# Asking for the next step's columns before the step's piece of w1, in a linear-attention and mixture-of-experts kernel

## The reference

```python
for t in range(S):                              # attention, B=4, H=8, S=768, D=48
    cur = einsum('bhd,bhe->bhde', u * k_t, v_t)
    y[:, :, t] = einsum('bhd,bhde->bhe', r_t, state + cur)
    state = w * state + einsum('bhd,bhe->bhde', k_t, v_t)
...
logits = x @ phi                                # mixture: x is 3072 x 384, 32 slots, 8 experts
slot_input = softmax_over_tokens(logits).T @ x
h = maximum(slot_input[e] @ w1[e], 0); slot_out[e] = h @ w2[e]      # w1[e] 384 x 1024
x = softmax_over_slots(logits) @ slot_out
...
h = x @ w_in; g = h * sigmoid(1.702 * h); out = g @ w_out           # 384 -> 2048 -> 384
```

## Time and profile before

| | |
|---|---|
| median of 3 runs | 385.01 us (383.77 to 385.17) |
| the profiled execution | 383.42 us, span 381.6 us |
| TensorE's granted clock | 0.999 of full |
| busy: TensorE, VectorE, ScalarE, POOL | 371.2, 233.2, 186.6, 98.2 us |
| DMA moved | 63.57 MB |
| attention stage | about 7 to 121 us |
| loop, chunks 1 to 4, on SyncE | 18.6 to 89 us |

### The profile page before, as it was taken

One profiled execution on the slowest core, in us unless ns is written; L12 is line 12 of the kernel. 1 busy time (PEld: TensorE's weight loads), 2 busy tenths in 40 slices (PEclk: granted clock), 3 DMA queues, 4 the chain that ended last, 5 costly groups with the idle time before them and its releaser, 6 DMA issues.

```text
span 381.6 us, 9077 instructions
## 1 busy us (share of the span) xinstructions
PE 371.2 (97%) x3198; PEld 290.7 (76%) x3198; DVE 233.2 (61%) x431; ACT 186.6 (49%) x398; POOL 98.2 (26%) x114
## 2 busy tenths in 40 slices
PE   6989999999999999999999999999999999999996
PEld 5877787877876344487888888888888888888885
DVE  8958697877783201687755556555555555555550
ACT  1234454445445241668565546455645564465451
POOL 6998888888671100100000000000000000000000
PEclk9999999999999999999999999999999999999999
DMA  7789999999999999600020002000200020002002
GB/s 287 269 313 395 398 391 397 400 392 375 391 336 413 342 394 413 254 0 2 1 82 3 0 2 82 0 0 0 82 0 0 0 82 0 0 5 78 0 2 82
DMA packets 21655, 63.57 MB, mean 167 GB/s; under 512 B 3073, under 2 KB 6674, under 8 KB 21250
## 3 DMA queue, kind: packets, MB, share of 16 engines
q1 hardware_dynamic: 20864, 63.09, 43.3%
q10 hardware_dynamic: 770, 0.19, 0.2%
HBM read 58.55 MB, written 4.72 MB: 166 GB/s over the span
## 4 chain that ended last, share of the span: by engine, by line
PE 94%; POOL 2%; DMA 2%; issue 1%; ACT 1%; DVE 0%; POOLq 0%; DVEq 0%; ACTq 0%
PE bank L651 11%; PE bank L653 11%; PE bank L652 11%; PE bank L392 6%; PE pair L651 6%; PE pair L652 6%; PE pair L653 6%; PE pair L441 6%; PE bank L638 4%; PE pair L429 3%; PE pair L412 3%; PE bank L600 3%; PE bank L462 3%; PE bank L580 2%; PE bank L471 2%; PE bank L453 2%
## 5 line engine op out<-in xcount | busy, mean ns | idle before, releaser
L946 DVE TENSOR_TENSOR gf<-bank,sg 128x512 f32<-128x512 f32 x72 | 49.8, 691 | 58.2 <-ACT sg L1155 58.0
L1155 ACT ACTIVATE sg<-bank 128x512 f32<-128x512 f32 x72 | 42.9, 598 | 70.6 <-PE bank L638 70.6
L651 PE MATMUL bank<-glo,whi 128*128 128x512 f32 x190 | 73.9, 389 | 0.0
L653 PE MATMUL bank<-ghi,wlo 128*128 128x512 f32 x190 | 73.9, 389 | 0.0
L652 PE MATMUL bank<-ghi,whi 128*128 128x512 f32 x190 | 73.9, 389 | 0.0
L957 DVE TENSOR_TENSOR glo<-gf,ghi 128x512 fp32r<-128x512 f32 x96 | 66.3, 691 | 0.3
L1161 ACT ACTIVATE ghi<-gf 128x512 fp32r<-128x512 f32 x95 | 59.4, 625 | 1.8 <-DVE gf L946 1.7
L652 PEld LDWEIGHTS bank<-ghi,whi 128*128 128x128 f32 x190 | 35.7, 188 | 7.4
L653 PEld LDWEIGHTS bank<-ghi,wlo 128*128 128x128 f32 x190 | 35.7, 188 | 7.4
L651 PEld LDWEIGHTS bank<-glo,whi 128*128 128x128 f32 x190 | 35.7, 188 | 7.4
L789 DVE TENSOR_TENSOR rks<-rkb,bank 112x512 f32<-112x512 f32 x48 | 30.8, 683 | 12.1 <-PE pair L429 7.1
(11 more groups left out here) (183 smaller groups left out, 510.4 us busy)
## 6 DMA issues: line engine op xcount, KB each, us to landing
ring<-w SPq DMA_DIRECT2D x24, 512.0 KB, 5.9
rkb<-rk SPq DMA_DIRECT2D x23, 512.0 KB, 5.9
krb<-kr SPq DMA_DIRECT2D x24, 384.0 KB, 5.0
ring<-w SPq DMA_DIRECT2D x4, 1536.0 KB, 13.8
ring<-w SPq DMA_DIRECT2D x8, 768.0 KB, 9.1
vb<-v SPq DMA_DIRECT2D x24, 192.0 KB, 5.0
out<-ob SPq DMA_DIRECT2D x18, 256.0 KB, 2.1
ring<-win SPq DMA_DIRECT2D x3, 1024.0 KB, 15.7
```

Of the source, the lines that this page charges most:

```text
L651: pe.matmul(o, w_hi, lo, start=(f == 0), stop=False)
L653: pe.matmul(o, w_lo, hi, start=False, stop=(f == KF - 1)).then_inc(prod_ps, 1)
L946: dve.tensor_tensor(gf[:, f % 2, :], bank[f % 4][:, :], sg[:, f % 2, :], ALU.mult).then_inc(gf_ok, 1)
L1155: act.activation(sg[:, f % 2, :], bank[f % 4][:, :], ACT.Sigmoid, scale=1.702).then_inc(sg_ok, 1)
```

## The change

In SyncE's `step` the line that asks for the next step's columns stands before the line that asks for the pieces of w1. Nothing else changes: the same requests, waits and buffers, and every other engine has the same instructions in the same order.

```diff
                 load_kr(c, b)
                 load_v(c, b)
-                load_w1(first, count)
                 if not (is_last(c) and b == B - 1):
                     load_rk(*following(c, b))
+                load_w1(first, count)
```

## The result

The change makes the kernel slower by a little: 386.23 us median of 14 runs (384.54 to 387.28) against 384.31 us for the kernel before, 14 runs taken beside them (383.34 to 386.26). The ratio is 1.0040, with a 95% interval of 1.0022 to 1.0058; that is +0.8 to +2.2 us, while the two medians are 1.9 us apart. I had forecast no change, with 385.0 us. The measured median lies within the stated range, but the two kernels differ beyond their scatter, and the forecast of no change is wrong.

A forecast was written before the change was run, and what follows sets the result against it. TensorE was taken to bound the loop, with the DMA close behind. The terms rk, w1, kr and dry queue summed to 0 (bounds -2.6 and about +0.5), giving a median of 385.0 us, range 383.4 to 386.6.

The forecast's parts named there:

- TensorE bounds the loop; the DMA has 0.75 us to spare a chunk: Attention loop, chunk 2: TensorE needs 18.65 us, the DMA 17.9 us for 7.08 MB at 396 GB/s.
- rk's issue does not move, it lands 1.3 us earlier, and no wait for it was on the path: Steady loop: rk still waits for VectorE's buffer, one w1 piece less lies ahead; gain 0, bounded by 2.6 us.
- w1 later costs 0 by itself: Loop: a w1 piece goes out some 2 us later; 14 us of cover before TensorE reads w1, cost 0.
- The issue of kr just fits: Step with two w1 pieces: kr could issue at 90.35, its buffer came free at 90.46; cost 0 to 0.1 us on SyncE.
- In the queue kr has the same bytes ahead of it as before, so it lands as before, provided that the queue never ran dry: Loop requests behind rk and w1: kr's landing stays unchanged if the queue never empties; cost 0.
- 0.2 us in all, bounds 0 and 0.5: Transfer time lost in the loop: a few dry moments of about 0.1 us each while w1 is held.
- My test: Thinnest loop step: v lands at 85.87, rk is in effect at 85.8, so not dry by less than 0.1 us.
- 1.9 us of delay: Time before a DMA request counts: kr on a nearly idle queue landed after 2.9 us, less 1.0 us of transfer.
- Who pays: the last weights, w_out: After the loop, about 155 us: lost transfer time reaches w_out; 0.56 us of slack, so even 0.5 us costs 0.
- Rival 2: Loop: queue runs dry behind the wait for rks, transfers bind, kr late; +6 us, 391 us; chance 0.06.
- The weighed rule: Loop DMA: at the skill's 358 GB/s a chunk would need 19.8 us and be transfer-bound; set aside for the measured rows.
- The instruction stall: Chunk 1, before 30.80: TensorE stops 0.88 us without a semaphore; might move, 384.1 to 385.9 us, chance 0.08.

## Why the prediction was wrong

- *TensorE bounds the loop; the DMA has 0.75 us to spare a chunk.* The bound is right, shown by the kernel without w1 in the loop: the same chunk times to 0.1 us. The spare of 4% was all the room there was, and a held w1 takes more than that.
- *rk's issue does not move, it lands 1.3 us earlier, and no wait for it was on the path.* The waits for rk went, and gained nothing. The size was off: 0.4 us earlier at the median.
- *w1 later costs 0 by itself.* Right: nobody waits for w1.
- *The issue of kr just fits.* Missed: 0.45 us late in the fourth step, where I had allowed 0.1, and not hidden by slack of POOL, which waits for that kr. No run puts a price on this part alone.
- *"In the queue kr has the same bytes ahead of it as before, so it lands as before, provided that the queue never ran dry", and "0.2 us in all, bounds 0 and 0.5".* This is the step that failed. The landings show about 1 us lost in the fourth step of each of chunks 2 to 4, 3.6 us over their twelve steps, against 0.2 us for the whole kernel in the forecast; that is 1.2 a chunk, more than the 0.75 of reserve. (Going by the rates comes to a like 2.8 us, 56.9 us against 21.3 MB at 393 GB/s, but this is only the longer chunk told in other words.) My test had two faults. It looked at one step and called it the thinnest, while the fourth steps were as thin: v issued at 67.43 lands at 72.1, and the rk of 70.29 with 1.9 us of delay counts from 72.2. And it asked whether rk arrives before v has landed, as if the queue were one thing. In the changed kernel the fourth step passes this test with 1 us to spare (v lands at 74.4, rk of 71.44 counts from 73.3), and the time is lost all the same, a little later, between rk and w1, with part of the engines without a packet (share 0.68 at 75.2 to 75.8). What is shown is that this comes with the hold and that kr pays for it; why engines stand empty with requests issued is not.
- *Who pays: the last weights, w_out.* Wrong payer. In the profile of the changed kernel ScalarE does not wait for w_out at all. POOL pays, for kr, and I had not followed the loop in which it pays: kr late, POOL late, VectorE's sum and scaling late, the wait for rks longer (14.8 to 19.6 us), w1 held longer.
- *Rival 2* named the mechanism and its deciding point (0.19 us dry a step; measured 1.2 a chunk by the landings, 0.3 a step), and expected +6 us at 0.5 a step, with a smaller loss of 2 us included. Measured is +1.5 to +1.9. It was the right account, and had a chance of 6%. The row that should have raised it was in hand: a thinnest step with less than 0.1 us to spare.
- *The weighed rule.* The page "DMA: Bandwidth & Descriptors" of the Trainium skill gives 358 GB/s; the rows of both kernels are above it (361 to 399), so it stays no bound here. At the 374 GB/s of the changed kernel 7.08 MB take the 18.9 us that chunks 3 and 4 now last, but that holds for any kernel whose loop moves its bytes in its own time, and does not show that the transfers' rate was the bound.
- *The instruction stall* stayed in place, 0.75 us where it was 0.88.
- *The median within the range* is no merit of the forecast. The range was made for scatter and for the stall; a loss of 1.5 to 1.9 us by a mechanism that was given 0.06 happens to fit into it.

## What to carry to other kernels

In a loop whose transfers have only a few per cent to spare, as here, a request that waits for nothing belongs ahead of a request that must wait, not behind one, even if nobody needs its data soon. Whatever stands behind a waiting request in an in-order issuer inherits the wait, and the request after it too. Where order seems to matter, look first for the buffer that makes the requests wait: with four kr buffers in place of two this kernel gains 1.3 to 1.6 us (383.03 and 383.12 us against 384.63 and 384.38), and with four of both (382.67 and 382.61 us) no difference between the orders can be measured.

## What the runs showed of the hardware

Averaged over a chunk, a DMA share near 1 says nothing on whether anybody waits: 0.99 to 1.01 went with the slower chunks of the changed kernel, 1.00 and 377 GB/s with chunks at TensorE's floor. In stretches of half a microsecond to one it falls where engines are short of packets (0.68 and 0.78, against 0.95 and 0.97 before). And in every profile with w1 in the loop, in both orders, the DMA falls to about half its rate for some 3 to 5 us early in chunk 5, somewhere between 102 and 113 us (before: 202 GB/s at share 1.03 from 105 to 107); the requests for w2 aren't its cause, and what is stays open.
